# A delta-rule attention fused with two MLP layers: chunk 0 computed without a state

## The chip, the cores and the metric

The kernel runs on one core of a Trainium2 chip. The metric is the device time of one execution in microseconds (us). The kernel before takes 1042.99 us, the median of three runs (1042.28 to 1044.95).

## The reference

```python
for t in range(S):                       # attention: B=4, H=8, S=768, D=48
    kt, vt, bt = k_n[:, :, t], v[:, :, t], beta[:, :, t, None]
    y[:, :, t] = einsum('bhd,bhde->bhe', q[:, :, t], state)      # reads the state before the step
    v_old = einsum('bhde,bhd->bhe', state, kt)
    state = state + bt[:, :, :, None] * einsum('bhd,bhe->bhde', kt, vt - v_old)
x = y as (B*S, H*D)                      # 3072 tokens x 384
h = x @ w_in;  x = softplus(h) @ w_out   # 384 -> 2048 -> 384
h = x @ w_in2; out = (h * cos(h)) @ w_out2
```

`k_n` are the keys divided by their norms. All in float32.

## The kernel before

**Tiles and chunks.** The 768 steps of a sequence are cut into 12 steps of 64 tokens (`C`), and two steps make a chunk, so there are 6 chunks (`NCH`). The 32 pairs of batch and head are held as 16 units in each half of the partitions. One chunk of attention gives 512 tokens, which is one tile `t` of the first MLP. Large products split each float32 operand into a rounded high part and the remainder (`x_hi`, `x_lo`, `wi_hi`, `wi_lo`) and add up three products (L1388 to L1390, L1412 to L1414).

**Attention in a chunk.** For each step the kernel needs the inverse of a unit lower triangular 64x64 matrix, built from the products of the keys. It is made by forward substitution on 32x32 diagonal blocks (31 rounds of two instructions) and then merged: `merge_inner` (jobs M1, L1145) and `merge_outer` (F1, L1157) on TensorE. `solve_values` (V0, V1, L1190) applies the inverse to the values, VectorE's `take_delta` scales the result with beta into `delta`. `add_to_state` (SN0, SN1, L1203) makes the step's share of the state from keys and `delta`, `keys_on_state` (KS0, KS1, L1171) gives what the state already holds for the next step's keys, which VectorE's `take_rest` subtracts from the values, and `read_out` (Y0, Y1) adds queries on state (L1220) and masked scores on `delta` (L1226). `turn_out` (YT0, YT1, L1248) transposes the result into `x_hi`/`x_lo`. Chunk 0 goes through all of these too, with a state of zeros.

**Who does the substitution.** For chunk 0 VectorE does it (`first_solve`, L894 and L897). For every later chunk GpSimd does it (`scale_blocks` L430, `clean` L424, `substitute` L440 and L443). GpSimd's `scale_blocks(1)` starts when VectorE's `take_diagonal(1)` (L796, L803) has turned the blocks of chunk 1:

```python
pool.wait_ge(blk_set, blocks_until(c))       # scale_blocks, c = 1: four increments
...
take_inner(0, 1)                             # VectorE, first(), before
take_diagonal(1)
dve.wait_ge(consts_set, 3)
mask_scores()
take_delta(0, 0, "V0")
```

The finished inverse of chunk c is picked up by VectorE's `take_inverse(c)` (L912, L914), which waits on `inv_ready`.

**The order of the work.** `begin()` and `first()` of each engine do chunk 0 and preparations for chunk 1, written out by hand. Then comes the fused stage: for each `ft` of the 16 column blocks of a tile, TensorE runs `product1(n+1)`, one piece of the next chunk's `attention` generator, `product2(n)`, and another piece. VectorE does a piece, `main(n+1)` (L1036, L1043, L1045: it gives the `g_hi`, `g_lo` that `product2(n+1)` waits for), and a piece. Each engine works strictly in its own order. In VectorE's `attention(1)` the seventh piece is `take_inverse(1)`, and it stands directly ahead of `main(4)`:

```python
next(jobs)                                   # VectorE, ft = 3: take_inverse(1)
main(t * FT + ft + 1)                        # main(4)
next(jobs)
```

On TensorE `product2(4)` waits for `main(4)` (`g_ready`), and all that follows on TensorE stands behind it.

Intermediate results of attention pass through a ring of three PSUM banks (`spare`); contents are numbered in the order of the table `FIRST` for chunk 0 and `ORDER` afterwards, and `taken[n % 3]` tells that a bank has been read out. SyncE issues the loads in written order, each behind a semaphore.

Of the kernel before, what the change touches and what calls it, by code (L numbers as in the profile page):

```python
# [13 lines left out]
P = 128  # L14
# [84 lines left out]
def build(nc, ctx, q, k, v, beta, pieces1, pieces2, x2, out):  # L99
# [12 lines left out]
    wi_hi, wi_lo = (sb(n, [P, FT, KT, P], F32R) for n in ("wi_hi", "wi_lo"))  # L112
    wo_hi, wo_lo = (sb(n, [P, FT, DM], F32R) for n in ("wo_hi", "wo_lo"))
# [64 lines left out]
    beta_loaded, q_loaded, v_loaded = sem("beta_loaded"), sem("q_loaded"), sem("v_loaded")  # L178
    k_loaded = [sem(f"k_loaded{i}") for i in range(4)]
# [32 lines left out]
    def diagonals(c, need):  # L212


        return need if c == 0 else 8 + 4 * (c - 1) + need

# [22 lines left out]
    def place(n):  # L239
        return spare[n % 3]  # L240
# [41 lines left out]
    def _(sp):  # L282
# [23 lines left out]
        def load_v(g):  # L306
            for h in range(2):
                sp.dma_start(res_v[C * h:C * h + C, :, :], rows(v, h, g)).then_inc(v_loaded, 16)
# [27 lines left out]
        load_v(0)  # L336
        load_piece(STAGE1, stage1, w1_loaded, pieces1, 2)
        sp.wait_ge(filled, cid(0, "Q0", 1) + 1)
        load_q(1)
        sp.wait_ge(w_split, 1)  # L340
        load_piece(STAGE1, stage1, w1_loaded, pieces1, 3)
        sp.wait_ge(filled, cid(0, "V0", 1) + 1)
        load_v(1)
        sp.wait_ge(filled, cid(0, "SN0", 1) + 1)
        load_k(4)
        sp.wait_ge(filled, cid(0, "V1", 1) + 1)
        load_v(2)
        sp.wait_ge(filled, cid(0, "Q1", 1) + 1)
        load_q(2)
# [152 lines left out]
    def _(act):  # L502
# [32 lines left out]
        def take_scores():  # L535
            for o in range(2):
                n = cid(0, "P0", o)
                act.wait_ge(filled, n + 1)
                copy(pT[:, o::2, :], place(n)[:, :].rearrange("p (a t) -> p a t", t=C)).then_inc(taken[n % 3], 1)
# [22 lines left out]
        def take_y(c, job):  # L562
            for o in range(2):
# [3 lines left out]
                     place(n)[:, 0:PAIRS * D].rearrange("p (a e) -> p a e", e=D)).then_inc(taken[n % 3], 1)  # L567

# [53 lines left out]
        def first():  # L622
            take_transposes(0, "Q0", qT)
            take_scores()
            take_transposes(1, "T0", knT[:, fill_of(1, 0)])
            take_transposes(1, "T1", knT[:, fill_of(1, 1)])
# [10 lines left out]
            take_transposes(0, "Q1", qT)  # L637
            take_x(0, 0, "YT0")
            take_y(0, "Y1")
            take_x(0, 1, "YT1")  # L640
            high_weights(3)
            square(2)

        def attention(c):
            after = c + 1 < NCH
            if 1 < c < NCH - 1:
                root(c + 1)
# [129 lines left out]
    def _(dve):  # L777
# [36 lines left out]
        def take_rest(c, s, job):  # L814
            dve.wait_ge(v_loaded, 32 * (2 * c + s + 1))
# [638 lines left out]
```

## Time and profile before

| | |
|---|---|
| three runs | 1042.28, 1042.99, 1044.95 us |
| the profiled execution | 1042.99 us, its span 1041.0 us |
| TensorE busy | 989.5 us, 95% of the span |
| VectorE busy | 729.8 us, 70% |
| ScalarE busy | 505.5 us, 49% |
| GpSimd busy | 324.7 us, 31% |
| first product of the fused stage starts | 88.12 us |

Times below are counted from the start of the span. A timeline row gives the start, the time that the group took (or that one took), engine, source line, operation, operands and count. A bracket at its end gives the idle time of the engine before it and who ended it. On TensorE a float32 matmul of attention shows as two records, so 32 matmuls read "x64"; the 128x128 transposes show as one each. A granted clock of 0.50 is 1.2 GHz, of 1.00 is 2.4 GHz.

### The profile page before, as it was taken

The page shows a single profiled execution, that of the slowest core. Times are in us where ns is not written, and L with a number is a line of the kernel's source. Part 1 is how long each engine was busy: PE and PEld are TensorE (multiplying, and loading weights), DVE is VectorE, ACT ScalarE, POOL GpSimd, SP SyncE. Part 2 cuts the span into 40 slices and gives each one's busy share as a digit, 9 for nine tenths or more (in the row PEclk, how much of TensorE's full clock was granted, in tenths as well). Part 3 has the DMA queues.
Part 4 walks back from the last instruction along what each step waited for, and adds up shares of the span by engine and source line. Part 5 has one row for each costly group of instructions (what it writes and reads, how often), then busy time and mean ns, then how long its engine had stood idle before and what let it go on. Part 6 is the DMA issues. An engine that isn't in the chain of part 4 may idle for free.

```text
span 1041.0 us, 26077 instructions
## 1 busy us (share of the span) xinstructions
PE 989.5 (95%) x11416; PEld 847.6 (81%) x11416; DVE 729.8 (70%) x1094; ACT 505.5 (49%) x813; POOL 324.7 (31%) x383
## 2 busy tenths in 40 slices
PE   4587999999999999999999999999999999999997
PEld 3476878788878888887788887999999999999996
DVE  5945875768586768755654897777777777687775
ACT  3534653563455355344535535545455445454443
POOL 2099358802950691186000673100101001010000
PEclk8659999999999999999999999999999999999999
DMA  8033213102110310011004411002020020000101
GB/s 186 18 71 71 78 48 63 47 2 48 32 47 19 62 46 3 18 33 47 18 2 140 140 55 61 1 1 61 1 58 4 1 61 1 15 16 1 31 1 31
DMA packets 100704, 42.66 MB, mean 41 GB/s; under 512 B 76496, under 2 KB 95952, under 8 KB 100592
## 3 DMA queue, kind: packets, MB, share of 16 engines
q1 hardware_dynamic: 96320, 40.12, 15.3%
q8 instruction: 90, 1.47, 0.6%
q10 hardware_dynamic: 4272, 0.89, 0.5%
q14 instruction: 22, 0.18, 0.1%
HBM read 31.56 MB, written 9.44 MB: 39 GB/s over the span
## 4 chain that ended last, share of the span: by engine, by line
PE 88%; DVE 7%; ACT 2%; issue 1%; DMA 0%; SPq 0%; DVEq 0%; ACTq 0%
PE wide L1388 9%; PE wide L1390 8%; PE wide L1389 8%; PE wide L1413 4%; PE wide L1414 4%; PE wide L1412 4%; PE bank L1389 4%; PE bank L1390 4%; PE bank L1388 4%; PE wide L1408 3%; PE wide L1410 3%; PE wide L1409 3%; PE bank L1410 3%; PE bank L1409 3%; PE bank L1408 3%; PE bank L1412 3%
## 5 line engine op out<-in xcount | busy, mean ns | idle before, releaser
L1388 PE MATMUL wide<-x_hi,wi_hi 128*128 128x512 f32 x408 | 167.2, 410 | 1.5 <-DVE x_lo L845 1.5
L1045 DVE TENSOR_TENSOR g_lo<-tmp,g_hi 128x512 fp32r<-128x512 f32 x192 | 160.0, 833 | 6.6
L1390 PE MATMUL wide<-x_hi,wi_lo 128*128 128x512 f32 x408 | 161.0, 395 | 0.0
L1389 PE MATMUL wide<-x_lo,wi_hi 128*128 128x512 f32 x408 | 160.8, 394 | 0.0
L725 ACT ACTIVATE tmp<-wide 128x512 f32<-128x512 f32 x88 | 52.6, 598 | 205.8 <-PE wide L1390 205.7
L1036 DVE SCALAR_TENSOR_TENSOR tmp<-wide,tmp 128x512 f32<-128x512 f32 x88 | 60.6, 688 | 123.2 <-ACT tmp L729 122.9
L443 POOL TENSOR_TENSOR inv<-inv,blk 128x31 f32<-128x31 f32 (+15 forms) x155 | 116.5, 752 | 12.2
L1043 DVE CAST g_hi<-tmp 128x512 fp32r<-128x512 f32 x192 | 103.4, 539 | 20.1 <-DVE tmp L1036 0.9
L470 POOL TENSOR_TENSOR x_lo<-x_raw,x_hi 128x1536 fp32r<-128x1536 f32 x6 | 23.5, 3910 | 273.1 <-ACT x_hi L504 273.1
L1026 DVE TENSOR_SCALAR tmp<-tmp 128x512 f32<-128x512 f32 x96 | 55.1, 574 | 69.2 <-ACT tmp L716 69.2
L440 POOL TENSOR_TENSOR blk<-blk,inv 128x31 f32<-128x31 f32 (+15 forms) x155 | 93.0, 600 | 12.4
L1388 PEld LDWEIGHTS wide<-x_hi,wi_hi 128*128 128x128 f32 x408 | 77.4, 190 | 16.9 <-issue 1.7
L1390 PEld LDWEIGHTS wide<-x_hi,wi_lo 128*128 128x128 f32 x408 | 77.0, 189 | 16.9
L1389 PEld LDWEIGHTS wide<-x_lo,wi_hi 128*128 128x128 f32 x408 | 77.3, 190 | 12.8
L716 ACT ACTIVATE tmp<-wide,consts 128x512 f32<-128x512 f32 x48 | 33.1, 689 | 99.5 <-PE wide L1390 99.5
L1413 PE MATMUL wide<-g_lo,wo_hi 128*128 128x512 f32 x192 | 74.9, 390 | 0.0
L1414 PE MATMUL wide<-g_hi,wo_lo 128*128 128x512 f32 x192 | 74.9, 390 | 0.0
L1412 PE MATMUL wide<-g_hi,wo_hi 128*128 128x512 f32 x192 | 74.9, 390 | 0.0
L716 ACT ACTIVATE tmp<-bank,consts 128x512 f32<-128x512 f32 x48 | 33.0, 687 | 79.9 <-PE bank L1390 79.9
L734 ACT ACTIVATE tmp<-tmp,consts 128x512 f32<-128x512 f32 x96 | 69.8, 727 | 3.1
L1390 PE MATMUL bank<-x_hi,wi_lo 128*128 128x512 f32 x168 | 66.3, 395 | 0.0
L1389 PE MATMUL bank<-x_lo,wi_hi 128*128 128x512 f32 x168 | 66.2, 394 | 0.0
(139 smaller groups left out, 2187.0 us busy)
## 6 DMA issues: line engine op xcount, KB each, us to landing
stage<-in_moe_w_in SPq DMA_DIRECT2D x32, 192.0 KB, 3.4
stage<-in_moe_w_out SPq DMA_DIRECT2D x8, 768.0 KB, 5.2
qn<-in_q SPq DMA_DIRECT2D x24, 192.0 KB, 3.7
res_v<-in_v SPq DMA_DIRECT2D x24, 192.0 KB, 3.6
x_t<-x_res SPq DMA_DIRECT2D x6, 768.0 KB, 3.6
x_raw<-x_t SPq DMA_DIRECT2D x6, 768.0 KB, 6.3
out_x<-res SPq DMA_DIRECT2D x24, 192.0 KB, 3.0
kn<-in_k SPq DMA_DIRECT2D x40, 96.0 KB, 3.0
```

The source lines that it names most:

```text
L440: nc.gpsimd.tensor_tensor(prod, blk[:, j + 1:BLK, j:j + 1].to_broadcast(shape), inv[:, j:j + 1, 0:j + 1].to_broadcast(shape), ALU.mult).th ...
L443: nc.gpsimd.tensor_tensor(inv[:, j + 1:BLK, 0:j + 1], inv[:, j + 1:BLK, 0:j + 1], prod, ALU.subtract).then_inc(inv_ready if j == BLK - 2 e ...
L716: nc.scalar.activation(tmp[ring(n)][:, :], bank[4 + ring(n)][:, :], ACT.Identity, bias=consts[:, 0:1], scale=INV_2PI).then_inc(rounded, 1)
L734: nc.scalar.activation(t, t, ACT.Sin, bias=consts[:, 1:2], scale=-2 * math.pi).then_inc(act_step, 1)
L1043: nc.vector.tensor_copy(hi, g).then_inc(g_hi_set, 1)
L1045: nc.vector.tensor_tensor(lo, g, hi.bitcast(FP32), ALU.subtract).then_inc(g_ready, 1)
L1388: mm(dst, wi_hi[:, ft, kt, :], hi[:, kt, :], start=(kt == 0), stop=False)
L1389: mm(dst, wi_hi[:, ft, kt, :], lo[:, kt, :], start=False, stop=False)
L1390: last = mm(dst, wi_lo[:, ft, kt, :], hi[:, kt, :], start=False, stop=(kt == KT - 1))
L1412: mm(dst, wo_hi[:, ft, cols], hi[:, :], start=first, stop=False)
L1413: mm(dst, wo_hi[:, ft, cols], lo[:, :], start=False, stop=False)
L1414: last = mm(dst, wo_lo[:, ft, cols], hi[:, :], start=False, stop=final)
```

## The change

In chunk 0 the state starts from zero, so its second step is expressed without one. New products of keys and queries with the first step's keys (jobs K1, `key_cross`, and X1, `query_cross`; function `cross`) are made early. KS1 becomes `key_cross` on the first step's deltas, Y0 becomes masked scores on deltas alone, Y1 becomes `query_cross` on `delta_0` plus `late_pT` on `delta` in two further banks (`acc[1:3]`), and the state after chunk 0 is made in one piece at the end (`first_state`). P1 and Q1 move ahead of the merges. SN0 goes away, KS0 of chunk 1 stays. The step-0 and step-1 values, deltas and the output of the second step get buffers of their own, laid over the second halves of `wi_lo` and `wo_lo`, which are written later. The masks become two VectorE products on SBUF. `keep_warm` puts 28 products of `ident` with `ident`, 128x128 each, whose result nobody reads, between the products of the chain: 18 once the substitution has reached `first_step` 50, then 1, 2, 2, 1, 1, 1 and 2. The `diagonal_gram` calls of chunk 1 move between the merges, and VectorE's `take_diagonal(1)` moves behind `take_delta(0, 1, "V1")`. `square(2)` and `reduce(2)` move into chunk 1's generator. SyncE loads the second step's values early, and loads `k` of step 4 behind `first_state`.

```diff
-FIRST = ("Q0", "P0", "T0", "T1", "S1", ("M1", 0), ("M1", 1), ("F1", 0), "V0", ("F1", 1), "SN0", "KS1", "Y0", "V1", "Q1",
-         "SN1", "P1", "YT0", "Y1", "YT1")
+FIRST = ("Q0", "P0", "K1", "T1", "Q1", "P1", "X1", "T0", "S1", ("M1", 0), ("M1", 1), ("F1", 0), "V0", ("F1", 1), "KS1", "Y0",
+         "V1", "YT0", "SN1")
...
         def first():                                   (VectorE)
             take_inverse(0)
             turn_inverse(0)
             take_inner(0, 0)
             take_inner(0, 1)
+            dve.wait_ge(consts_set, 3)
+            take_delta(0, 0, "V0")
+            mask_scores("P0", pT)
+            take_rest(0, 1, "KS1")
+            mask_scores("P1", late_pT)
+            take_delta(0, 1, "V1")
             take_diagonal(1)
-            dve.wait_ge(consts_set, 3)
-            mask_scores()
-            take_delta(0, 0, "V0")
-            take_state(0, 0, "SN0")
-            take_rest(0, 1, "KS1")
-            take_delta(0, 1, "V1")
+            take_x(0, 0, "YT0")
+            take_late_x()
             take_state(0, 1, "SN1")
-            take_p(0, "P1")
-            take_x(0, 0, "YT0")
-            take_x(0, 1, "YT1")
             low_weights(2)
...
+        def keep_warm(times):
+            for _ in range(times):
+                mm(acc[0][:, 0:P], ident[:, :], ident[:, :], start=True, stop=True)
...
             gram(1, 1)                                 (TensorE)
             pe.wait_ge(blanked, 3)
+            pe.wait_ge(first_step, 2 * 25)
+            keep_warm(18)
             merge_inner(0, 0)
             merge_inner(0, 1)
+            diagonal_gram(1, 0)
+            keep_warm(1)
             merge_outer(0, 0)
+            diagonal_gram(1, 1)
+            keep_warm(2)
             solve_values(0, 0, "V0")
             merge_outer(0, 1)
-            add_to_state(0, 0, "SN0")
-            keys_on_state(0, 1, "KS1")
-            read_out(0, 0, "Y0")
+            keep_warm(2)
+            await_pair(pe, cid(0, "V0"))
+            on_deltas(room_for("KS1"), key_cross, delta_0, filled)
+            pe.wait_ge(scores_masked, 1)
+            on_deltas(room_for("Y0"), pT, delta_0, filled)
+            keep_warm(1)
             solve_values(0, 1, "V1")
-            pe.wait_ge(q_loaded, 64)
-            transposes(0, "Q1", qn)
-            add_to_state(0, 1, "SN1")
-            scores(0, 1)
+            on_deltas(acc[1:3], query_cross, delta_0, out_filled, final=False)
+            keep_warm(1)
+            await_pair(pe, cid(0, "V1"))
+            pe.wait_ge(scores_masked, 2)
+            on_deltas(acc[1:3], late_pT, delta, out_filled, first=False)
             turn_out(0, "YT0", "Y0")
-            read_out(0, 1, "Y1")
-            turn_out(0, "YT1", "Y1")
+            keep_warm(2)
+            turn_late()
+            first_state()
```

VectorE, chunk 0 after the substitution, in the kernel before (L796 and L803 are `take_diagonal(1)`, L827 `take_delta`, L836 `take_state`, L819 `take_rest`, L845 `take_x`):

```order
L926 COPY inv<-bank 32x512 x4
L796 STREAM_TRANSPOSE beta_blk<-beta_t 128x32
L803 STREAM_TRANSPOSE blk<-wide 128x1024
L931 SCALAR_TENSOR_TENSOR pT<-mask,pT 128x1024
L827 TENSOR_TENSOR delta<-bank,beta_key 128x8x48 x2
L836 TENSOR_TENSOR state<-state,bank 128x384 x2
L819 TENSOR_TENSOR res_v<-res_v,bank 128x8x48 x2
L827 TENSOR_TENSOR delta<-bank,beta_key 128x8x48 x2
L836 TENSOR_TENSOR state<-state,bank 128x384 x2
```

The same place with the change (L839 and L846 are `take_diagonal(1)`, L871 `take_delta`, L982 the masks, L863 `take_rest`):

```order
L977 COPY inv<-bank 32x512 x4
L871 TENSOR_TENSOR delta<-bank,beta_key 128x8x48 x2
L982 TENSOR_TENSOR pT<-pT,mask 128x1024
L863 TENSOR_TENSOR res<-res,bank 128x8x48 x2
L982 TENSOR_TENSOR late_pT<-late_pT,mask 128x1024
L871 TENSOR_TENSOR delta<-bank,beta_key 128x8x48 x2
L839 STREAM_TRANSPOSE beta_blk<-beta_t 128x32
L846 STREAM_TRANSPOSE blk<-wide 128x1024
L889 TENSOR_TENSOR x_lo<-bank,x_hi 128x3x128 x2
L896 TENSOR_TENSOR x_lo<-wide,x_hi 128x3x128 x2
L880 TENSOR_TENSOR state<-state,bank 128x384 x2
```

`take_diagonal(1)` has moved from directly behind the merges' copies to behind the second step's deltas, eight instructions later.

VectorE further on, in the fused stage with the change (L1087, L1094, L1096 are `main`, L928 `reduce(2)`, L934 `low_weights(3)`, L963 and L965 `take_inverse(1)`):

```order
L918 TENSOR_TENSOR kn<-kn,norm 128x32x48
L834 SCALAR_TENSOR_TENSOR pT<-mask,bank 128x8x64 x2
L1087 SCALAR_TENSOR_TENSOR tmp<-wide,tmp 128x512
L1094 CAST g_hi<-tmp 128x512
L1096 TENSOR_TENSOR g_lo<-tmp,g_hi 128x512
L963 STREAM_TRANSPOSE blk<-inv 128x32x32
L965 TENSOR_TENSOR blk<-blk,beta_t 128x1024
L1087 SCALAR_TENSOR_TENSOR tmp<-wide,tmp 128x512
L1094 CAST g_hi<-tmp 128x512
L1096 TENSOR_TENSOR g_lo<-tmp,g_hi 128x512
```

This piece stands as it did before: `take_inverse(1)` between `main(3)` and `main(4)`. GpSimd's instructions are the same, in the same order.

## Rows read from the trace of the kernel before

**Rows 1.** The page: TensorE's busy tenths over 40 slices of 26 us

```profile
PE   4587999999999999999999999999999999999997
```

**Rows 2.** TensorE's timeline in the chain of chunk 0 (start, us, ...)

```profile
52.12 3.72 PE L1145 MATMUL bank<-blk,aT 32*32 32x32 f32 x128 [7.45 <-DVE blk L914]
...
88.12 0.77 PE L1388 MATMUL wide<-x_hi,wi_hi 128*128 128x512 f32 x1 [1.51 <-DVE x_lo L845]
```

**Rows 3.** Stretches: length, busy PE, PEld, DVE, ACT, POOL, clock, DMA share, GB/s

```profile
52.10:77.20 25.10, 21.02 (x648) 19.97 (x648) 11.25 (x16) 8.81 (x15) 22.68 (x27) 0.50 0.30 67
77.50:87.50 10.00, 6.47 (x268) 5.53 (x268) 3.99 (x8) 3.59 (x8) 9.06 (x13) 1.00 0.60 117
```

**Rows 4.** VectorE's timeline, end of the substitution and chain of chunk 0

```profile
54.14 1.39 DVE L926 COPY inv<-bank 32x512 f32<-32x512 f32 x2 [0.25 <-PE bank L1145]
...
57.37 0.21 DVE L796 STREAM_TRANSPOSE beta_blk<-beta_t 128x32 f32<-128x32 f32 x1
57.61 1.25 DVE L803 STREAM_TRANSPOSE blk<-wide 128x1024 f32<-128x1024 f32 x1
58.79 1.22 DVE L931 SCALAR_TENSOR_TENSOR pT<-mask,pT 128x1024 f32<-128x1024 f32 x1
...
75.57 1.02 DVE L827 TENSOR_TENSOR delta<-bank,beta_key 128x384 f32<-128x384 f32 x2 [6.73 <-PE bank L1190]
```

**Rows 5.** GpSimd's timeline, chunk 1: scaling, clearing, first and last substitution, slow ones

```profile
58.94 3.28 POOL L430 TENSOR_TENSOR blk<-blk,beta_blk 128x1024 f32<-128x1024 f32 x1
62.80 0.95 POOL L424 MEMSET inv<- 128x1024 f32 x1 [0.57 <-PE bank L1157]
...
64.05 0.25 POOL L440 TENSOR_TENSOR blk<-blk,inv 128x31 f32<-128x31 f32 x1
...
86.18 0.85 POOL L443 TENSOR_TENSOR inv<-inv,blk 128x255 f32<-128x255 f32 x1
...
87.83 2.44 POOL L443 TENSOR_TENSOR inv<-inv,blk 128x252 f32<-128x252 f32 x1
...
101.66 1.89 POOL L440 TENSOR_TENSOR blk<-blk,inv 128x156 f32<-128x156 f32 x1
103.63 0.61 POOL L443 TENSOR_TENSOR inv<-inv,blk 128x156 f32<-128x156 f32 x1
...
108.22 1.72 POOL L443 TENSOR_TENSOR inv<-inv,blk 128x60 f32<-128x60 f32 x1
...
110.35 0.27 POOL L443 TENSOR_TENSOR inv<-inv,blk 128x31 f32<-128x31 f32 x1
```

**Rows 6.** GpSimd's scaling over all five chunks (min/median/max ns)

```profile
L430 POOL TENSOR_TENSOR blk<-blk,beta_blk x5: 2374/2377/3282, 58.9 to 440.5; 128x1024 f32<-128x1024 f32 x5
```

**Rows 7.** VectorE's timeline in the fused stage

```profile
87.78 1.75 DVE L883 TENSOR_TENSOR wi_lo<-stage,wi_hi 128x1536 fp32r<-128x1536 f32 x1
...
112.70 2.16 DVE L912 STREAM_TRANSPOSE blk<-inv 128x1024 f32<-128x1024 f32 x1
```

**Rows 8.** TensorE's timeline at 2.4 GHz: product2(4), M1, solve_values, transposes, diagonal products

```profile
118.82 0.47 PE L1412 MATMUL bank<-g_hi,wo_hi 128*128 128x512 f32 x1
...
121.04 2.21 PE L1145 MATMUL bank<-blk,aT 32*32 32x32 f32 x128
...
134.83 1.15 PE L1190 MATMUL bank<-res_v,aT 64*64 64x48 f32 x64
```

**Rows 9.** The same view, earlier

```profile
37.06 1.89 PE L1131 MATMUL wide<-knT 48*32 48x32 f32 x192
...
110.35 1.03 PE L1085 MATMUL bank<-ident,kn 128*128 128x128 f32 x8
```

**Rows 10.** The chain in order of time (start, us): product1(0) around the clock's rise

```profile
90.59 0.43 PE wide L1390
...
91.36 0.23 PE wide L1389
```

**Rows 11.** ScalarE's timeline in the chain of chunk 0

```profile
57.64 1.19 ACT L504 ACTIVATE aT<-bank 32x512 f32<-32x512 f32 x2 [1.12 <-PE bank L1157]
```

More of the change, by code:

```diff
@@ L336, in _ @@
         load_v(0)
+        load_v(1)
         load_piece(STAGE1, stage1, w1_loaded, pieces1, 2)
@@ L339, in _ @@
         load_q(1)
+        sp.wait_ge(filled, cid(0, "Q1", 1) + 1)
+        load_q(2)
         sp.wait_ge(w_split, 1)
@@ L846, in take_x, with take_late_x @@
                                         x_hi[c % 2][:, :, at:at + P].bitcast(FP32), ALU.subtract).then_inc(taken[n % 3], 1)
+        def take_late_x():
+            for bb in range(2):
+                at = 256 + bb * P
+                dve.wait_ge(xh_set, 3 + bb)
+                nc.vector.tensor_tensor(x_lo[0][:, :, at:at + P], acc[1 + bb][:, 0:DM].rearrange("p (k t) -> p k t", t=P),
+                                        x_hi[0][:, :, at:at + P].bitcast(FP32), ALU.subtract).then_inc(out_taken, 1)
         def factors(c):
@@ L1253, in keys_transposed, with cross @@
             transposes(c, "T1" if s else "T0", kn[:, (2 * c + s) % 4])
+        def cross(job, right):
+            n = cid(0, job)
+            await_room(pe, n)
+            await_room(pe, n + 1)
+            for a in range(PAIRS):
+                for o in range(2):
+                    for h in range(2):
+                        rows = slice(Q2 * o, Q2 * o + D)
+                        last = mm(place(n + o)[key_half(h, o), a * C:a * C + C], knT[rows, fill_of(0, 0), a, key_half(h, o)],
+                                  right(rows, a, h, o), start=True, stop=True)
+                    if a == PAIRS - 1:
+                        last.then_inc(filled, 1)
@@ new lines, in other_keys, with other_queries, on_deltas @@
+        def other_keys(rows, a, h, o):
+            return knT[rows, fill_of(0, 1), a, key_half(h, o)]
+        def other_queries(rows, a, h, o):
+            return qT[rows, a, C * h:C * h + C]
+        def on_deltas(out, left, right, done, first=True, final=True):
+            for a in range(PAIRS):
+                for o in range(2):
+                    for h in range(2):
+                        at = key_half(h, o)
+                        last = mm(out[o][C * h:C * h + C, a * D:a * D + D], left[at, 2 * a + o, :], right[at, 2 * a + o, :],
+                                  start=first and a == 0, stop=final, skip_group_check=True)
+                    if final and a == PAIRS - 1:
+                        last.then_inc(done, 1)
@@ new lines, in room_for, with first_state @@
+        def room_for(job):
+            n = cid(0, job)
+            await_room(pe, n)
+            await_room(pe, n + 1)
+            return place(n), place(n + 1)
+        def first_state():
+            out = room_for("SN1")
+            for s in range(2):
+                for a in range(PAIRS):
+                    for h in range(2):
+                        for o in range(2):
+                            at = key_half(h, o)
+                            last = mm(out[h][Q2 * o:Q2 * o + Q2, a * D:a * D + D], kn[at, s, 2 * a + o, :],
+                                      values_of(0, s)[1][at, 2 * a + o, :], start=s == 0 and a == 0, stop=s == 1,
+                                      skip_group_check=True)
+                        if s and a == PAIRS - 1:
+                            last.then_inc(filled, 1)
+                if s == 0:
+                    last.then_inc(from_state, 1)
@@ L1255, in begin, with turn_late @@
+        def turn_late():
+            pe.wait_ge(out_taken, 2)
+            for bb in range(2):
+                for kt in range(KT):
+                    at = bb * DM + kt * P
+                    last = nc.tensor.transpose(acc[1 + bb][:, kt * P:kt * P + P], y_late[:, at:at + P], ident[:, :])
+                last.then_inc(out_filled, 1)
+        def keep_warm(times):
+            for _ in range(times):
+                mm(acc[0][:, 0:P], ident[:, :], ident[:, :], start=True, stop=True)
         def begin():
```

117 lines of the change are left out of this document (77 added, 40 removed).

## The prediction

> **What bounds the kernel now.** I read the page first. TensorE is busy 95% of the span, and its row over 40 slices shows where it isn't: the first three slices, some 80 us [rows 1]. Behind them TensorE runs nearly without gaps, so a change in chunk 0 is worth what it moves the fused stage. TensorE's timeline shows the chain there: the merges start at 52.12, when VectorE has the inverse, and the first product of the fused stage at 88.12, that is 36.0 us later [rows 2]. The stretches show that from 52.1 to 77.2 the clock is at 0.50 (1.2 GHz) and from 77.5 at 1.00 [rows 3]; TensorE had been idle for 7.45 us before 52.1 [rows 2].
>
> The view that decides is GpSimd's. Its work for chunk 1 starts at 58.94, as soon as VectorE has turned the blocks (57.61 + 1.25), and its last substitution ends at 110.35 + 0.27 = 110.62 [rows 4, 5]. VectorE picks this inverse up at 112.70 [rows 7], only 2.1 us later. `main(4)` stands behind that pick-up, and `product2(4)` on TensorE starts at 118.82 [rows 8], 6.12 us after the pick-up began. So GpSimd's 52 us are the second longest chain of the head, hidden with 2.1 us to spare.
>
> **The head with the change, at 2.4 GHz.** VectorE's substitution and so 52.12 don't move. The early products (K1, Q1, P1, X1) run on TensorE while VectorE substitutes. The 18 unread products are two records of the size of a transpose each, 1.03/8 = 0.13 us [rows 9], so 18 x 2 x 0.13 = 4.7 us at 2.4 GHz, and twice that at 1.2. They fill the time before 52.1 that was idle [rows 2], and I take it that the chain then starts at 2.4 GHz. Prices there: M1 2.21 for both, F1 half of it, each product set of attention 1.15 [rows 8], a diagonal product set 256 records at 1.89/192, thus 1.26 [rows 9], an unread product 0.26.
> - M1 52.1 to 54.3. VectorE turns the inverse until 53.9 (54.14 less 0.25 idle), then copies twice 1.39: 55.4 and 56.8 [rows 4].
> - TensorE: diagonal products and one unread product to 55.9, F1 to 57.0. ScalarE writes it out in 1.19 to 58.2 [rows 11]. Diagonal products and two unread ones end at 58.7.
> - V0 58.7 to 59.9, deltas 1.02 to 61.0, first mask 1.22 to 62.2, KS1 61.5 to 62.6, rest 1.02 to 63.7, second mask to 64.9. V1 64.0 to 65.1, deltas to 66.2 [rows 4, 8].
> - Only now `take_diagonal(1)`: 0.2 + 1.25, done at **67.7** instead of 58.9.
> - The second step's output (66.7 to 67.8), its copy (to 68.7), transposes (to 69.9), `x_lo` (to 71.3) and the state (to 72.2) let the fused stage start at **72.2** instead of 88.1. It would also start at 2.4 GHz, where before seven 0.43 us products came ahead of the 0.23 us ones [rows 10], worth 7 x 0.2 = 1.4. The head gains 15.9 + 1.4 = 17.3 us.
>
> **What is late next.** GpSimd scales in 2.4 (median of five; the 3.28 before lay beside VectorE's mask [rows 5, 6]), clears and starts 62.80 to 64.05 = 1.25, and substitutes for 110.62 - 64.05 = 46.6 us [rows 5]. The inverse of chunk 1 is there at 67.7 + 2.4 + 1.25 + 46.6 = **117.9**, instead of 110.6. VectorE comes to it at 112.7 - 17.3 = 95.4 and stands for some 22 us. `main(4)` is queued behind it, so is `product2(4)`. TensorE can still finish `product1(5)`, then it has nothing. `product2(4)` starts at 117.9 + 6.2 = 124.1, against 118.82: **+5.3 us**. All that the head gained is spent in this wait, and more.
>
> TensorE will have been idle some 20 us, so the clock is at 1.2 GHz on return, as it was after the idle time before 52.1 [rows 2, 3]. The nearest row for the way back is the start of the fused stage: seven slow products, +1.4 us; no row says how the return runs at this place, so the bounds are 0 and twice this. Behind 124 the program is as before and TensorE's queue is full, so nothing gives this back. Sum: 5.3 + 1.4 = +6.7 us on the profiled execution's 1042.99, which is also the median of the runs: **1049.7**.
>
> Costed at nothing: the later root of chunk 2, `square(2)`, the loads moved on SyncE (second values early, `k` of step 4 behind the state's first half at 71), and the ScalarE copies of K1, P1 and X1. Their cover is the substitution at 29 to 49 or the 22 us wait; were that wait gone, the k loads and the norms of chunk 2 could cost a us or two each. The shorter chain's fewer products are covered by the same wait.
>
> **Bounds of the GpSimd stage.** Three of its instructions took 2.44, 1.89 and 1.72, where one of the size of the first takes 0.85 and one of the second's 0.61 [rows 5]; the first lies beside VectorE's 1.75 us split of weights [rows 7]. If the long wait of VectorE leaves GpSimd alone and none of this returns (1.6 + 1.3, and at most 1.3 for the third, which is smaller than the second), the substitution is 46.6 - 4.2 = 42.4 us and the sum +2.5. If all return it is 46.6. I take 46.6, since the weight splits and the key scaling that lie beside them come before the pick-up in VectorE's order, and so still lie in GpSimd's stretch.
> The Trainium skill, "SBUF — State Buffer", on the shared port pair, says that a VectorE instruction with two SBUF inputs and a GpSimd instruction that reads SBUF exclude each other for the whole of the one that came first. By that rule the same instructions lock GpSimd out again and the sum stays at +6.7; without it the 42.4 would be as good a guess. The 2.44 us row agrees with it.
>
> **Rivals.**
> 1. *The clock stays or falls to 1.2 GHz in the chain.* For: the row of 52.1 to 77.2 shows 84% busy TensorE and no rise. Against: the low clock followed idle time, which is now filled, and from 77.5 to 87.5 it held at 1.00 with TensorE only 65% busy [rows 3]. If it is low throughout, M1 takes 3.72 for 2.21 [rows 2, 8] and every other set 1.7 times as long too, and the same walk ends the turned blocks at 77.1: +9.4 more, 1059.1. A fall midway gives about half of it, 1054.
> 2. *GpSimd is quicker alone.* As bounded above: +2.5, 1045.5.
> 3. *The gain comes through: faster.* The mechanism would be that the pick-up of chunk 1's inverse doesn't hold `main(4)`. Then TensorE keeps the 17.3 us: 1042.99 - 17.3 = 1025.7. It decides by the time the inverse is ready: it must be there before 118.82 - 6.2 = 112.6 for any gain, and before 95.4 for all. Against it: even if all waits for TensorE vanished, VectorE's own instructions from 53.9 (2.78, 1.02, 1.22, 1.02, 1.22, 1.02, 1.46 [rows 4]) end the turned blocks at 63.6, and with 50.2 the inverse at 113.8. Only a much quicker GpSimd stage beats that.
> 4. *The unread products delay the merges.* At 1.2 GHz 18 of them take 9.4 us; begun at 45.5 they end at 54.9, 2.8 us late: 1052.5. The preceding work from 32 to 47 has few gaps, so I think the clock is up by then.
>
> **Numbers.** Forecast 0.66, its own range 1047 to 1052. Rival 1 0.16, rival 4 alone 0.05, rival 2 0.07, rival 3 0.04; 0.02 for what I don't see. The range takes in rival 2 and the half of rival 1: 1045 to 1056. 0.3% is 3.1 us, about what a measurement of this kernel can tell from no change; rival 2 and the forecast's lowest edge fall within it, 0.10. Faster 0.05, slower 0.85.
>
> **What would show it.** In the profile of the changed kernel: VectorE idle some 22 us ahead of the transpose of `inv` in `take_inverse(1)`, put down to GpSimd; TensorE idle about 20 us ahead of `product2(4)`, starting near 124; GpSimd scaling from about 67.7, its last substitution at about 118; the first `product1` near 72; the clock at 1.00 from 52 to 95. I am wrong if that idle time of VectorE is under 5 us, or if GpSimd's stage is under 45 us. A first product later than 75 speaks for rivals 1 or 4.

## The result, and the profile after

| | median of the runs | runs | profiled execution | its span |
|---|---|---|---|---|
| before | 1043.97 us (1042.28 to 1045.76) | 4 | 1042.99 us | 1041.0 us |
| changed | 1063.05 us (1061.87 to 1069.67) | 4 | 1063.38 us | 1061.7 us |

The changed kernel is slower: the ratio is 1.0196, with a 95% interval from 1.0149 to 1.0242. The forecast was 1049.7 us with a range of 1045 to 1056. The direction is right. The size is not: the loss is nearly three times the one forecast, and it lies outside the range.

The page of the changed kernel, in the rows that answer to [rows 1]: busy us of TensorE, then its busy tenths and its clock in 40 slices.

```profile
PE 998.0 (94%) x11534; PEld 853.8 (80%) x11534; DVE 732.4 (69%) x1091; ACT 508.6 (48%) x819; POOL 324.7 (31%) x383
PE   4879389999999999999999999999999999999997
PEclk8759789999999999999999999999999999999999
```

TensorE was busy for 989.5 of 1041.0 us before and is busy for 998.0 of 1061.7 now. So 8.5 us of the 20.7 are more work or slower work, and 12.2 us are more idle time. The idle time lies at the start of the span: slice 5 (106 to 133 us) has fallen to 3 tenths. The forecast wait is there. This is VectorE's timeline at the pick-up of chunk 1's inverse, the place of [rows 7]:

```profile
131.50 2.02 DVE L963 STREAM_TRANSPOSE blk<-inv 128x1024 f32<-128x1024 f32 x1 [19.24 <-POOL inv L469]
```

And TensorE's, which answers to `product2(4)` at 118.82 and M1 at 121.04 in [rows 8]:

```profile
137.44 0.77 PE L1541 MATMUL bank<-g_hi,wo_hi 128*128 128x512 f32 x1 [20.18 <-DVE g_lo L1096]
...
141.55 1.64 PE L1196 MATMUL bank<-blk,aT 32*32 32x32 f32 x78
```

`product2(4)` is 18.6 us later than before, and M1 20.5 us. That is the whole difference; behind it the two programs run alike. The forecast had +5.3 and +6.7 here. GpSimd's rows show that its stage is not what was mis-sized (to compare with [rows 5]):

```profile
80.92 2.37 POOL L456 TENSOR_TENSOR blk<-blk,beta_blk 128x1024 f32<-128x1024 f32 x1 [22.32 <-DVE blk L846]
...
84.47 0.26 POOL L466 TENSOR_TENSOR blk<-blk,inv 128x31 f32<-128x31 f32 x1
...
131.21 0.27 POOL L469 TENSOR_TENSOR inv<-inv,blk 128x31 f32<-128x31 f32 x1
```

The substitution takes 131.48 - 84.47 = 47.0 us; 46.6 were forecast. It only begins late: the blocks are turned at 80.84, where 67.7 was forecast. The error lies in TensorE's chain in front of it, so that is the view to read. TensorE's timeline of the changed kernel from the unread products to the first product of the fused stage (start, us, line, tiles, count, and in brackets the idle time ahead with what ended it; "issue" means that the engine waited for nothing that the profile shows):

```profile
48.07 4.29 PE L1366 MATMUL bank<-ident 128*128 128x128 f32 x36
52.28 2.21 PE L1196 MATMUL bank<-blk,aT 32*32 32x32 f32 x128
54.42 0.29 PE L1182 MATMUL wide<-knT 48*32 48x32 f32 x15
55.53 1.16 PE L1182 MATMUL wide<-knT 48*32 48x32 f32 x113 [0.81 <-issue]
56.62 0.68 PE L1366 MATMUL bank<-ident 128*128 128x128 f32 x2
57.22 0.53 PE L1208 MATMUL bank<-aT,inv 32*32 32x32 f32 x12
60.99 1.60 PE L1208 MATMUL bank<-aT,inv 32*32 32x32 f32 x52 [3.24 <-issue]
62.52 1.05 PE L1182 MATMUL wide<-knT 48*32 48x32 f32 x76
64.44 0.79 PE L1182 MATMUL wide<-knT 48*32 48x32 f32 x52 [0.86 <-issue]
...
66.31 1.96 PE L1240 MATMUL bank<-res_v,aT 64*64 64x48 f32 x64
...
86.00 0.50 PE L1517 MATMUL wide<-x_hi,wi_hi 128*128 128x512 f32 x1
```

The start is as forecast: 36 records of unread products in 4.29 us, M1 at 52.28 in 2.21 us, at 2.4 GHz where [rows 2] show 3.72. Then TensorE stands for 0.81, 3.24 and 0.86 us. Each of these stalls lies inside a set (15 + 113, 12 + 52, 76 + 52 records), and inside a set the program has no wait. The sets behind them take 1.96 us where 1.15 was reckoned. The stretches of the same kernel, to compare with [rows 3] (length, busy PE, PEld, DVE, ACT, POOL, clock, DMA share, GB/s):

```profile
40.00:56.50 16.50, 12.74 (x496) 11.66 (x494) 15.50 (x31) 12.61 (x19) 4.75 (x2) 1.00 0.16 29
57.00:80.50 23.50, 18.59 (x589) 16.88 (x588) 6.24 (x10) 5.73 (x10) 1.60 (x1) 0.50 0.19 53
137.40:142.00 4.60, 4.56 (x25) 3.27 (x27) 4.46 (x6) 1.54 (x2) 0.00 (x0) 0.50 0.61 173
```

The clock is at 1.00 through M1 and the first stall. It falls at 56.8, ahead of the 3.24 us stall, and is at 0.50 (1.2 GHz) from 57 to 80.5, which is rival 1. The head gains 2.1 us (86.00 for 88.12), not 15.9.

### The profile page after: what moved, and what is told of

Read it like the earlier page. It is cut to its first block, busy times and chain, and to the rows that moved or that the text cites. A ratio compares the mean times of both kernels' runs of the same rounds, so it can differ in the third digit from the quotient of the medians.

```text
span 1061.7 us, 26312 instructions
## 1 busy us (share of the span) xinstructions
PE 998.0 (94%) x11534; PEld 853.8 (80%) x11534; DVE 732.4 (69%) x1091; ACT 508.6 (48%) x819; POOL 324.7 (31%) x383
## 3 DMA queue, kind: packets, MB, share of 16 engines
q8 instruction: 91, 1.49, 0.6%
## 4 chain that ended last, share of the span: by engine, by line
PE 85%; DVE 5%; POOL 4%; ACT 2%; issue 2%; DMA 0%; SPq 0%; DVEq 0%; POOLq 0%
PE wide L1517 9%; PE wide L1519 8%; PE wide L1518 8%; PE bank L1518 4%; PE bank L1519 4%; PE wide L1541 4%; PE wide L1543 4%; PE wide L1542 4%; PE bank L1517 4%; PE wide L1537 3%; PE wide L1539 3%; PE wide L1538 3%; PE bank L1539 3%; PE bank L1538 3%; PE bank L1537 3%; PE bank L1541 2%
## 5 line engine op out<-in xcount | busy, mean ns | idle before, releaser
L1096 DVE TENSOR_TENSOR g_lo<-tmp,g_hi 128x512 fp32r<-128x512 f32 x192 | 160.4, 836 | 6.6
L1087 DVE SCALAR_TENSOR_TENSOR tmp<-wide,tmp 128x512 f32<-128x512 f32 x88 | 60.6, 689 | 120.8 <-ACT tmp L772 120.6
L1094 DVE CAST g_hi<-tmp 128x512 fp32r<-128x512 f32 x192 | 104.8, 546 | 20.2 <-DVE tmp L1087 0.5
L1518 PEld LDWEIGHTS wide<-x_lo,wi_hi 128*128 128x128 f32 x408 | 76.8, 188 | 12.7
```

The lines of the kernel that those rows point to most:

```text
L1094: nc.vector.tensor_copy(hi, g).then_inc(g_hi_set, 1)
L1096: nc.vector.tensor_tensor(lo, g, hi.bitcast(FP32), ALU.subtract).then_inc(g_ready, 1)
L1518: mm(dst, wi_hi[:, ft, kt, :], lo[:, kt, :], start=False, stop=False)
```

## The theories put to the chip

- **A.** The place of `take_diagonal(1)` alone sets the loss: each us by which chunk 1's blocks are turned later is one by which `product2(4)` is later.
- **B.** The unread products cost more than they bring.
- **C1.** The "issue" stalls come from the 0.77 MB transfer of weights that SyncE sends off at 55.23. (The first of them, 54.71 to 55.53, lies ahead of it; C1 can only be about the other two.)
- **C2.** They come from the arrival of TensorE's own instructions, and would come whatever else moved.

What speaks for C2: in the changed kernel 113 + 2 + 12 = 127 records lie between the first and the second stall, and 52 + 76 = 128 between the second and the third. The page has a queue for instructions:

```profile
q8 instruction: 91, 1.49, 0.6%
```

That is 1.49 MB in 91 packets, 16 KB each. TensorE's 11534 matmuls, each with its weight load, divided by 128 give 90.1. The kernel before has 11416 and 90 packets (89.2); e6 has 11302 and 89 (88.3), e3 11480 and 90 (89.7). So one packet carries 128 matmuls with their weight loads (worked out from these counts; the trace has no row for a single packet's content). A float32 product of this kernel is two records (36 for 18). The Trainium skill, "Runtime: NRT & Kernel Launch", section "Instruction fetch mechanics", says the same of the size, 16 KiB blocks of 256 instructions that a queue of the sequencer's own brings while the block before runs, and calls the cost of a boundary mostly hidden. On the size the rows agree. On the cost they don't for this chain, as the experiments show.

## The experiments

**e2: the kernel before with the one edit.**

```diff
             take_inner(0, 1)
-            take_diagonal(1)
...
             take_delta(0, 1, "V1")
+            take_diagonal(1)
             take_state(0, 1, "SN1")
```

> The kernel before with only one edit: take_diagonal(1) behind take_delta(0, 1, V1). Theory A: the blocks are turned at about 76.6 + 1.45 = 78 instead of 58.9, the inverse is there 18 us later, near 128.5, product2(4) starts near 134.7, and with a slow restart the time is 1043 + 16 + 1.5 = 1060. Rival B: nobody waits, the time is within 2 us of before.

Measured: 1058.82 us (1058.67 to 1059.69) against 1043.53 for the kernel before, measured beside it, ratio 1.0149 (1.0134 to 1.0165). VectorE's and GpSimd's timelines:

```profile
75.65 1.21 DVE L803 STREAM_TRANSPOSE blk<-wide 128x1024 f32<-128x1024 f32 x1
127.55 2.02 DVE L912 STREAM_TRANSPOSE blk<-inv 128x1024 f32<-128x1024 f32 x1 [12.13 <-POOL inv L443]
```
```profile
76.94 2.36 POOL L430 TENSOR_TENSOR blk<-blk,beta_blk 128x1024 f32<-128x1024 f32 x1 [18.73 <-DVE blk L803]
```

One line moved down costs 15.3 us by itself. The blocks are turned 18.0 us later than in [rows 4] (76.86 for 58.86). `product2(4)` starts at 133.49, 14.7 us later: the rest went mostly on the 2.1 us that GpSimd had to spare and on its scaling, 2.36 us for the 3.28 of [rows 5]. Theory A holds. From the turned blocks to `product2(4)` it is 56.6 us in the change and 56.6 in e2 (59.96 in the kernel before, which had the spare time).

**e1: the change with the blocks early.** The diagonal products of chunk 1 stand ahead of the merges, `take_diagonal(1)` right behind the copies of M1, as before.

```diff
             gram(1, 1)                                 (TensorE)
+            for s in range(2):
+                diagonal_gram(1, s)
...
-            diagonal_gram(1, 0)
...
-            diagonal_gram(1, 1)
...
             take_inner(0, 1)                           (VectorE)
+            take_diagonal(1)
...
             take_delta(0, 1, "V1")
-            take_diagonal(1)
```

> The changed kernel with one part undone: the diagonal products of chunk 1 go back ahead of the merges and take_diagonal(1) back to directly behind take_inner(0, 1). Theory A (the wait for GpSimd's inverse of chunk 1 is what costs, because the blocks are turned late): GpSimd starts scaling near 58 again, the inverse is there near 110, VectorE's 19 us idle ahead of take_inverse(1) shrinks to under 5, and the time is 1040 to 1044. Rival B (the chain of chunk 0 itself, slowed by the 1.2 GHz clock and the 3.2 us stall, is what costs): the time stays within 3 us of the changed kernel's 1063.

Measured: 1053.12 us (1051.83 to 1058.26) against 1043.53, ratio 1.0102 (1.0073 to 1.0131). Ten of the 19 us are gone, not all. TensorE's timeline shows what came instead:

```profile
49.71 1.61 PE L1182 MATMUL wide<-knT 48*32 48x32 f32 x127 [1.52 <-issue]
53.60 1.05 PE L1182 MATMUL wide<-knT 48*32 48x32 f32 x76 [2.28 <-issue]
54.58 6.63 PE L1366 MATMUL bank<-ident 128*128 128x128 f32 x36
61.14 2.21 PE L1196 MATMUL bank<-blk,aT 32*32 32x32 f32 x128
```

The stalls are there again, in other instructions, 127 records apart. No load of weights bears on them: it leaves at 55.36 in this run, and the stretches of 2 us from 48 to 54 show a DMA share of 0.00 to 0.04. From one resumption to the next it is 3.89 us. The diagonal products end late and the unread ones behind them later still, so M1 starts at 61.14 and the blocks are turned at 66.80, 8 us later than before. The expectation of 1040 to 1044 failed in the first place because it took the diagonal products ahead of the merges to be free. GpSimd's stage adds to it: the clearing waits 1.30 us for F1 and the substitution takes 48.5 us (71.78 to 120.32), so that 59.5 us lie between the turned blocks and `product2(4)`.

**e3: the change without the unread products.** `keep_warm` returns at once.

> The changed kernel without its 28 unread products. If they only cost time in a chain that is at 1.2 GHz anyway (ten of them stand between its products): the blocks are turned some 4 us earlier than 80.8 and the time is 1057 to 1060. If they keep the clock up for a part of it (the merges ran at 2.4 GHz in the changed kernel): M1 takes 3.7 instead of 2.2, and the two about cancel, 1061 to 1064. If the 3.2 us stall inside F1 comes from where the instruction stream is cut, it moves or goes, for up to 3 us less.

Measured: 1065.37 us (1063.91 to 1066.96), ratio 1.0214 (1.0191 to 1.0237). This is just outside the 1061 to 1064 of the second guess, and the interval overlaps that of the change itself: no gain or loss can be told, and the table below shows why. M1 is at 1.2 GHz now. VectorE's timeline, then TensorE's:

```profile
50.51 1.23 DVE L965 TENSOR_TENSOR blk<-blk,beta_t 128x1024 f32<-128x1024 f32 x1
```
```profile
51.94 3.62 PE L1196 MATMUL bank<-blk,aT 32*32 32x32 f32 x128 [2.11 <-issue]
```

The bracket says "issue", but this idle time is not a stall of the kind above: M1 reads what VectorE writes at L965, and that ends at 51.74, 0.2 us ahead of M1. Two stalls inside sets are there as well, 1.03 us in F1 and 1.61 us in the diagonal products, and the records come again at 59.67 and 63.22, 3.55 us apart.

**e4: the change with the load of weights late.** Piece 3 leaves behind the second step's output; its high parts are made in chunk 1.

```diff
-        sp.wait_ge(w_split, 1)
-        load_piece(STAGE1, stage1, w1_loaded, pieces1, 3)
         sp.wait_ge(filled, cid(0, "V0", 1) + 1)
         load_v(2)
+        sp.wait_ge(out_filled, 2)
+        sp.wait_ge(w_split, 1)
+        load_piece(STAGE1, stage1, w1_loaded, pieces1, 3)
```

> The changed kernel with SyncE's load of weight piece 3 (0.77 MB, issued at 55.2 and in flight when TensorE stood still from 57.8 to 61.0 with no semaphore to wait for) moved behind the second step's output, and its rounding on ScalarE moved into chunk 1's generator. Theory C (TensorE waits there for its next instructions, whose fetch goes through the same DMA engines and stands behind the weights): the 3.2 us stall shrinks to about 0.8, as the one at 54.7, the clock may then stay at 2.4 GHz, and the blocks are turned between 68 and 77; time 1050 to 1059. Rival D (the stall has nothing to do with the load): it stays, time within 2 us of 1063.

Measured: 1063.83 us (1062.49 to 1068.67), ratio 1.0204 (1.0175 to 1.0233): no change. TensorE's timeline:

```profile
60.58 1.01 PE L1209 MATMUL bank<-aT,inv 32*32 32x32 f32 x52 [1.74 <-issue]
...
64.48 0.79 PE L1183 MATMUL wide<-knT 48*32 48x32 f32 x52 [1.97 <-issue]
```

The blocks are turned at 80.88, as in the change. The load leaves only at 81.23 here, and stalls of 1.74 and 1.97 us remain without it, so it is not what makes them. C1 falls. How much it adds is open. The stall in F1 has shrunk from 3.24 us, but TensorE also comes to it 1.1 us later, since M1 starts at 54.68 in this execution. Its records come at 60.58, where they came at 60.99 in the change. By that the load cost 0.4 us; by the distance between two resumptions (5.46 us from 55.53 to 60.99 in the change, 3.90 from 60.58 to 64.48 here) it would be 1.6.

M1 is 2.4 us late because the unread products ran at 1.2 GHz in part:

```profile
49.65 5.10 PE L1367 MATMUL bank<-ident 128*128 128x128 f32 x36
...
56.83 1.29 PE L1183 MATMUL wide<-knT 48*32 48x32 f32 x128
```

From there the clock holds at 1.00 up to 61.6, through the stall in F1, where it fell at 56.8 in the change. And still V0 starts at 66.35, against 66.31. So the records that TensorE waits for set this part of the chain, whatever the clock.

**e6: few records in place of many.** The 256 records of chunk 1's diagonal products between the merges give way to 24 products of one record each, of about the same time on TensorE. Chunk 1's blocks are left out by this, so its result isn't the right one; the order of the work is.

```diff
+        def stand_in():
+            pe.wait_ge(w_hi_set, 1)
+            for half in range(2):
+                for _ in range(3):
+                    mm(wide[1][:, 512 * half:512 * half + 384], wi_hi[:, 0, 0, :],
+                       wi_hi[:, 0, :, :].rearrange("p a b -> p (a b)"), start=True, stop=True)
+                    last = mm(wide[1][:, 512 * half + 384:512 * half + 512], wi_hi[:, 0, 0, :],
+                              wi_hi[:, 1, 0, :], start=True, stop=True)
+                last.then_inc(blocks_filled, 1)
...
-            diagonal_gram(1, 0)
+            stand_in()
...
-            diagonal_gram(1, 1)
+            stand_in()
```

> The changed kernel with the 256 records of chunk 1's diagonal products between the merges left out; in their place stand 24 products of 128x512 and 128x128 with one record each and the same TensorE time (1.3 us for each of the two sets). Chunk 1's inverse is not the right one. Theory C2: the stalls of TensorE behind M1 with no semaphore to wait for (0.8, 3.2 and 0.9 us in the changed kernel) shrink to under 1 us in all, since two blocks fewer have to come; the blocks are turned 4 to 9 us earlier than 80.8, and the time is 1054 to 1059. Rival D2 (the stalls come from the 0.77 MB load of weights or from something else at this time): a stall of 2 to 3 us stays near 57.8, and the time falls by 1 us at most.

Measured: 1058.45 us (1056.49 to 1060.42, two runs), ratio 1.0137 (1.0093 to 1.0181). TensorE's timeline and one stretch:

```profile
51.94 2.21 PE L1196 MATMUL bank<-blk,aT 32*32 32x32 f32 x128
...
56.22 1.20 PE L1208 MATMUL bank<-aT,inv 32*32 32x32 f32 x64
...
64.36 0.56 PE L1329 MATMUL bank<-delta,key_cross 64*64 64x48 f32 x22 [0.91 <-issue]
```
```profile
48.00:66.00 18.00, 16.36 (x477) 15.43 (x477) 11.64 (x16) 12.87 (x19) 6.89 (x2) 1.00 0.27 68
```

This is the decisive run. The load of weights is left where the change has it, and the busy time ahead is the same, but with 232 records fewer no stall is left before 63.4 us, and the clock holds at 1.00 up to 66, where it fell at 56.8 in the change. The merges and V0 run at the prices of the forecast (2.21, 1.20 and 1.15 us), and both the time and the blocks lie where C2 put them. C2 holds. The blocks are turned some 8.5 us earlier (GpSimd scales at 72.41), and `product2(4)` starts 8.4 us earlier. Yet the median fell by only 4.6 us; again the table below has the rest.

**e5 and e7: blocks early, and what then still binds.** e5 is e1 without the unread products.

> The changed kernel with the diagonal products and take_diagonal(1) back in their old places, and without the 28 unread products. In the run with the places restored the merges began only at 61.1, behind 18 unread products that could not start before 54.6. Theory C2 (TensorE's instructions arrive in blocks, 128 float32 records of a small product each, and at 2.4 GHz a block is used up before the next has come; what is put ahead of the merges pushes them): the merges start near 54.6, GpSimd begins its substitution 6 us earlier than there, and the time is 1045 to 1048, GpSimd's inverse still the last to come, by 1 to 3 us. Rival B2 (the unread products keep the clock up and are worth their place): the time is 1053 or more.

Measured: 1049.55 us against 1044.85, ratio 1.0055 (1.0037 to 1.0073), where e1 had 1.0102. That is 3.6 us better than e1 by the medians and 4.9 by the ratios, so B2 falls. It is 1.5 us above the range of the expectation and still slower than before. One of its eight executions took 1939 us and is left out of the ratio; it is the one that was profiled, so no trace of e5 is read. e7 is e5 with chunk 1's inverse in a buffer of its own, cleared at the start, and with `low_weights(0)` and `(1)` on VectorE:

```diff
         clean(0)                                       (GpSimd)
-        pool.wait_ge(invN_set, 1)
-        for n in range(2):
-            low_weights(n)
-        scale_blocks(1)
         clean(1)
+        scale_blocks(1)
         substitute(1)
...
             mask_scores("P0", pT)                      (VectorE)
+            low_weights(0)
...
             mask_scores("P1", late_pT)
+            low_weights(1)
```

> As the run with both (places restored, no unread products), and GpSimd's stage for chunk 1 shortened: the inverse of chunk 1 gets a buffer of its own over the second half of wo_hi, so it is cleared at the start and needn't wait for F1, and the remainders of weight pieces 0 and 1 (6.9 us on GpSimd) are made by VectorE in its idle time. GpSimd starts scaling as soon as the blocks are turned, near 59 to 60, and is done at 59.5 + 2.4 + 46.8 = 108.7. Theory A: the pick-up no longer waits or waits under 1 us, and the time is the head's alone, with the first product of the fused stage near 80 to 84 where before it was 88.1: 1038 to 1041. If VectorE's two splits (1.8 us each) fall on the chain of chunk 0, 2 to 4 us more.

Measured: 1050.55 us (1049.38 to 1054.4), ratio 1.0066 (1.0044 to 1.0089). It missed by 10 us. VectorE:

```profile
118.99 2.04 DVE L968 STREAM_TRANSPOSE blk<-inv_next 128x1024 f32<-128x1024 f32 x1 [7.75 <-POOL inv_next L477]
```

The head did not come as early as expected (first product of the fused stage at 85.56, not 80 to 84), and the pick-up waits 7.75 us. The blocks are turned at 64.06 and the substitution starts at 66.64, but it ends only at 118.96: 52.3 us, not 47. GpSimd and VectorE side by side show where most of the 5.3 us went:

```profile
69.43 1.80 POOL L477 TENSOR_TENSOR inv_next<-inv_next,blk 128x87 f32<-128x87 f32 x1
```
```profile
69.07 1.88 DVE L939 TENSOR_TENSOR wi_lo<-stage,wi_hi 128x1536 fp32r<-128x1536 f32 x1
```

Four GpSimd instructions lie beside VectorE's two masks and two splits of weights (67.71 to 75.25). They took 1.21, 1.80, 1.32 and 1.95 us; the same four took 0.35, 0.42, 0.47 and 0.57 in the change, where the masks and the splits lie ahead of the substitution or on GpSimd itself. That is 4.5 of the 5.3 us. Most of what moving the work off GpSimd saved came back as slower substitution.

**e8: one part of the change, in the kernel before.** 18 unread products in TensorE's 7.45 us wait ahead of M1 [rows 2].

```diff
             gram(1, 1)
+            n = cid(0, "M1", 0)
+            await_room(pe, n)
+            for _ in range(18):
+                mm(place(n)[:, 0:P], ident[:, :], ident[:, :], start=True, stop=True)
             pe.wait_ge(blanked, 3)
             merge_inner(0, 0)
```

> The kernel before with one part of the change alone: 18 products that nobody reads, put where TensorE waits for the blanked chain before the first merge (7.45 us without work in the profile before, 44.67 to 52.12). All else is the kernel before; the inverse of chunk 1 is as early as there (blocks turned at 58.9, GpSimd done at some 105.5) and so does not bind. If instructions come in blocks that can run ahead while TensorE idles or runs long products, the clock should be at 2.4 GHz when the merge starts, the merges and the first solves take 1.16 us a set where they took 1.96, up to the point at which the stock of instructions is used up; from there the clock falls and the sets are back at 1.96. In the chunk's chain of 52.12 to 88.12 I expect 3 to 6 us of gain and 1038 to 1041 us in all. If a chain of float32 sets at 2.4 GHz starves at once, the products cost nothing and bring nothing: 1043 to 1045. If they delay the first merge: 1045 to 1047, with the merge later than 52.1.

Measured: 1042.16 us (1039.59 to 1043.73, 10 runs) against 1044.36, ratio 0.9979 (0.9967 to 0.9991). TensorE:

```profile
44.86 6.13 PE L1283 MATMUL bank<-ident 128*128 128x128 f32 x36
52.88 2.21 PE L1145 MATMUL bank<-blk,aT 32*32 32x32 f32 x128 [1.88 <-issue]
...
88.37 0.77 PE L1392 MATMUL wide<-x_hi,wi_hi 128*128 128x512 f32 x1 [1.37 <-DVE x_lo L845]
```

M1 is at 2.4 GHz, but 0.76 us later than before. VectorE's product that it reads says why; here and in the kernel before:

```profile
51.55 1.23 DVE L914 TENSOR_TENSOR blk<-blk,beta_t 128x1024 f32<-128x1024 f32 x1
```
```profile
50.79 1.23 DVE L914 TENSOR_TENSOR blk<-blk,beta_t 128x1024 f32<-128x1024 f32 x1
```

VectorE itself is 0.76 us later in this execution, and it was 0.7 us later before the unread products began, so they did not delay M1, and the 1.88 us that the profile calls "issue" is a wait for VectorE. Behind M1 TensorE waits 1.15 us for VectorE's copies. In that wait, at 55.6, the clock falls to 1.2 GHz; the sets take 1.92 to 1.96 us again, and the fused stage starts at 88.37, against 88.12. From M1 on the chain is 35.5 us long, where it was 36.0: 0.5 us are gained, not the 3 to 6 that I expected. (The expectation also puts GpSimd's end at 105.5; in the kernel before it is 110.62 [rows 5]. It does not bind there either.) The median is 0.2% under that of before, with both bounds of the ratio below 1. It is the only kernel of this study under the time of before, but this trace, whose span is 1040.7 against 1041.0, doesn't show where the 2.2 us come from; that stays open.

## One sum that fits every trace

e3 and e6 look like contradictions: the inverse comes 3.5 and 8.4 us earlier than in the change, and the time does not follow. The missing part is how long TensorE runs at 1.2 GHz once it has something to do again. In e3 TensorE starts again at 133.92, behind 20.19 us of waiting. The stretch behind this start, and the same stretch of e6:

```profile
133.90:146.00 12.10, 12.08 (x148) 9.73 (x149) 7.38 (x10) 4.39 (x5) 0.00 (x0) 0.50 0.22 66
```
```profile
129.00:141.00 12.00, 11.95 (x148) 9.62 (x149) 7.41 (x10) 4.26 (x5) 0.00 (x0) 0.50 0.23 67
```

In both the clock stays at 0.50 for 12 us of nearly full work, in the change for 4.6. A stretch of full work at half the clock costs half its length. The table takes the start of `product2(4)` and the time at which the clock is back at 1.00 from each trace (the latter from stretches of 1 us); the last but one column is (start - 118.82) + (back - start) / 2.

| kernel | blocks turned | `product2(4)` starts | clock back | worked out | span - 1041.0 |
|---|---|---|---|---|---|
| change | 80.84 | 137.44 | 142.1 | +20.9 | +20.7 |
| e2 | 76.86 | 133.49 | 138.0 | +16.9 | +16.7 |
| e1 | 66.80 | 126.28 | 131.2 | +9.9 | +10.0 |
| e3 | 77.34 | 133.92 | 146.4 | +21.3 | +21.6 |
| e4 | 80.88 | 137.68 | 150.4 | +25.2 | +25.9 |
| e6 | about 72.3 | 129.05 | 141.7 | +16.6 | +17.7 |
| e7 | 64.06 | 124.93 | 128.1 | +7.7 | +6.0 |

Two numbers of one place give the span of seven kernels within 1.7 us, four of them within 0.3. What decides whether the return takes 3 or 12.7 us is not known from these runs: e2, e3 and e4 had idle times of 12.9, 20.2 and 16.9 us ahead and took 4.5, 12.5 and 12.7. e4's own profiled execution was its slowest (1068.67, its median 1063.83), which suggests that at that place the same kernel can fall either way; its other executions have no trace.

The table also tests theory A once more. From the turned blocks to `product2(4)` it is 56.6 to 56.8 us in the change, e2, e3, e4 and e6. Only e1 (59.5) and e7 (60.9) take longer, by the longer stages of GpSimd given above.

## Why the prediction was right or wrong

- **Right: the mechanism and its place.** VectorE stands at `take_inverse(1)` for 19.24 us (22 forecast) and TensorE ahead of `product2(4)` for 20.18 (20 forecast), as the section on what would show it said. e2 shows that the moved `take_diagonal(1)` is the edit that does it. Rival 3, that the gain comes through, is refuted.
- **Right: GpSimd's stage.** 46.6 us were taken and 47.0 measured; rival 2 falls. Its rows show the slow instructions again:

```profile
98.46 2.01 POOL L466 TENSOR_TENSOR blk<-blk,inv 128x231 f32<-128x231 f32 x1
```
```profile
97.77 2.23 DVE L934 TENSOR_TENSOR wo_lo<-stage,wo_hi 128x1536 fp32r<-128x1536 f32 x1
```

  The instructions of about this size took 0.6 us. By the rule that the prediction cited (the Trainium skill, "SBUF — State Buffer", the shared port pair), this is what it said, and the trace agrees.
- **Right: the unread products.** They fit into the wait and M1 started at 52.28 at 2.4 GHz, so rival 4 falls for this execution. Their price, 4.7 us, measured 4.29. But in e4, with the same products, the clock was at 1.2 GHz when they began, they took 5.10 us, and M1 was 2.4 us late, which is rival 4.
- **Wrong: "The head with the change, at 2.4 GHz", the walk from 54.3 to the blocks turned at 67.7.** It priced every set at its 2.4 GHz duration and laid them end to end, and so put the arrival of the records at nothing and the clock at 1.00 throughout. M1 ended at 54.5, as forecast. V0 then began at 66.31 and not at 58.7: 7.6 us, of which 4.9 are the three stalls and the rest mostly sets at 1.2 GHz. From V0 to the turned blocks it took 14.5 us and not 9.0: 5.5 us, without a stall, with every set at 1.2 GHz. Together this is +13.1 us on the one term that is passed on in full: 117.9 became 131.48, 124.1 became 137.44. (Rival 1's walk, 77.1, and the 3.24 us stall in F1 also add up to 80.3, near the 80.84 measured. That is luck in part: its walk has M1 at 3.72 us, which took 2.21.) How much of the 5.5 us would have come back at 2.4 GHz is open. In e6, with the clock up until 66.6 of 59.71 to 72.33, this stretch still took 12.6 us, with stalls of 0.91 and 0.26 in it.
- **A slip in the working:** a diagonal product set is 128 records and not 256; the 1.26 us that the walk uses is the price of 128, so the sum stands.
- **Wrong: the weight given to rival 1**, 0.16. Its 1059.1 was the nearest figure, and the range stopped at its half. The argument against it was that the low clock follows idle time, and the idle time was filled. It was filled in one place only; further idle time came from a cause that was not on the list. The stalls stood in the trace of before. The waits of TensorE from 20 to 50 us there (line, what it waited for: us in all, times, longest):

```profile
PE wide L1131 <- issue: 5.3, 2, 3.6
PE bank L1098 <- issue: 3.2, 2, 1.8
```

  and two of them in its timeline:

```profile
40.64 0.76 PE L1131 MATMUL wide<-knT 48*32 48x32 f32 x64 [1.69 <-issue]
41.36 1.15 PE L1098 MATMUL bank<-knT 48*64 48x64 f32 x63
44.31 0.36 PE L1098 MATMUL bank<-knT 48*64 48x64 f32 x1 [1.80 <-issue]
```

  These are 64 + 63 = 127 records, and 3.67 us from one resumption to the next. I read the 1.89 us for 192 records [rows 9] as a price and passed over the idle time in the rows beside it. Where 128 records need 3.7 us to arrive, a set of 64 at 2.4 GHz can't repeat every 1.15 us for long.
- **Nearly right: the return to 2.4 GHz behind the wait**, +1.4 forecast. It cost (142.1 - 137.44) / 2 = 2.3, within the bound of twice 1.4. In other kernels it cost up to 6.4, so that bound was too low in general.

Added up: 5.3 + 1.4 were forecast. Turned blocks 13.1 later, GpSimd 0.4 longer, the steps behind it 0.2 shorter and the return 0.9 dearer make 20.9, and 20.7 was measured in the span.

## What to carry to other kernels

When an instruction feeds a long stage on a slow engine that had 2 us to spare, moving it behind faster work costs its whole delay less those 2 us: follow the second longest chain before shortening the first. Before pricing a chain of small matmuls at the full clock, divide its records by the rate at which records arrive; "issue" rows inside a set, at even distances in records, are that rate, and fewer, larger products get past it where filler products don't, since these need records too. An "issue" row ahead of a set can be an ordinary wait, as M1's in e3 and e8 were: look at when the other engine's result was there. Price a restart after a wait like the ones here (7 to 20 us) with half of 3 to 12.7 us, not with the cheapest row at hand.

## What the runs showed of the hardware that I had not expected

- TensorE's instructions come in packets of 16 KB, each 128 matmuls with their weight loads, by the counts above. Stalls in a row resume 3.45 to 3.9 us apart (3.45 and 3.67 in the change and before, 3.89 in e1, 3.55 in e3, 3.9 in e4), and once 5.46 us apart with a 0.77 MB load beside them. At 1.2 GHz 128 records of M1 take 3.72 us, so M1 hides the arrival; at 2.4 GHz they take 2.21 and TensorE can run dry. The 128 records of a diagonal product set are shorter, 1.63 us even at 1.2 GHz in e3, and there stalls of 1.03 and 1.61 us show at that clock too. The Trainium skill's "mostly hidden" holds for the long products of this kernel and not for its small ones. A stock can be held ahead: in e4 M1 and the diagonal products, 256 records, ran through from 54.68 to 58.1 without one.
- The clock fell near such stalls: 1.3 us behind the first one in the change (56.8), behind the one in F1 in e4 (61.6). In e8 it fell at 55.6 in a wait for VectorE. Where it falls behind a stall the chain pays twice, once in idle time and then in slower sets; that the stall is what lowers it is read from the order alone, and no run separates it.
- The filler products raised the clock in e4 (at 51.4) and e8 (at 48.8), and M1 took 2.21 us behind them each time, 3.62 without them in e3. In the change, e1, e4 and e8 it fell again within 0.5 to 4.7 us of M1's end; in e6, with fewer records behind M1, it held for 12.5. With and without them the ratios are 1.0196 and 1.0214 in the change, 1.0102 and 1.0055 with the blocks early, 0.9979 and 1 in a wait of the kernel before: nothing that can be told, a loss, and a gain of 0.2%.
